# A delta-rule attention, a mixture of experts and a dense layer on one core: identities added by VectorE, weight splits and counts on GpSimd, the gate at the output's eviction, filler matmuls at two boundaries

## What is computed

```python
# attention: q, k, v of shape (4, 8, 768, 48), beta of shape (4, 8, 768)
k_n = k / (norm(k) + 1e-6)
for t in range(768):
    y[:, :, t] = q[:, :, t] @ state
    v_old = state.T @ k_n[:, :, t]
    state += beta[t] * outer(k_n[:, :, t], v[:, :, t] - v_old)
x = y, heads side by side                       # 3072 x 384
# mixture of experts, 8 experts, 1024 hidden
e = argmax(x @ w_gate); p = softmax(x @ w_gate)
out = p[e] * sigmoid(x @ w_output_gate)[e] * (relu(x @ w1[e]) @ w2[e])
# dense layer, 768 hidden
h = max(x @ w1, x @ w2, x @ w3); result = h @ w_out
```

## Time and profile before

| | us |
|---|---|
| median of three runs | 1106.98 (1105.72 to 1110.40) |
| the profiled execution | 1101.72 |
| its span in the profile | 1100.0 |
| TensorE busy | 1019.6 (93%) |
| VectorE busy | 519.5 (47%) |
| ScalarE busy | 366.4 (33%) |
| GpSimd busy | 311.3 (28%) |

### The profile page before, as it was taken

The page is one execution under the profiler, slowest core; times in us unless marked ns, Lnnn a source line. Parts: engine busy times, 40 slices in busy tenths (PEclk is TensorE's granted clock), DMA queues, the critical chain, the costliest instruction groups (busy, mean ns, idle before and its releaser), DMA issues. The chain is left out here.

```text
span 1100.0 us, 30946 instructions
## 1 busy us (share of the span) xinstructions
PE 1019.6 (93%) x13260; PEld 889.7 (81%) x13260; DVE 519.5 (47%) x1134; ACT 366.4 (33%) x731; POOL 311.3 (28%) x202
## 2 busy tenths in 40 slices
PE   4898998999999999849999999998699999999998
PEld 3787887888888888738999999997488888888888
DVE  5566666677666665425444444433342423233221
ACT  1455545455555555412222222221221222122111
POOL 3333242334233423015452555524400001000000
PEclk9999999999999999959999999999699999999999
DMA  9312112121212111045343445223201010100000
GB/s 304 122 34 65 55 41 73 55 72 41 72 56 72 41 45 34 16 172 177 100 149 134 172 172 172 79 86 122 65 22 44 15 44 16 48 18 18 19 11 29
DMA packets 58055, 84.90 MB, mean 77 GB/s; under 512 B 28880, under 2 KB 52816, under 8 KB 55376
## 3 DMA queue, kind: packets, MB, share of 16 engines
q1 hardware_dynamic: 52272, 46.94, 13.5%
q0 software_dynamic: 5664, 36.18, 9.7%
HBM read 61.67 MB, written 21.43 MB: 76 GB/s over the span
## 5 line engine op out<-in xcount | busy, mean ns | idle before, releaser
L1081 PE MATMUL hb<-early,last_h 128*128 128x512 f32 x648 | 207.8, 402 | 1.2 <-DVE early L1213 1.2
L1081 PEld LDWEIGHTS hb<-early,last_h 128*128 128x128 f32 x648 | 121.5, 190 | 29.3 <-DVE early L1213 1.6
L1081 PE MATMUL hb<-early,last_l 128*128 128x512 f32 x324 | 129.1, 399 | 0.0
L1219 DVE TENSOR_TENSOR m<-hb,m 128x512 f32<-128x512 f32 x36 | 24.9, 692 | 132.0 <-PE hb L1081 132.0
L329 PEld LDWEIGHTS bank<-t,n_hi 64*64 64x64 f16 x2688 | 65.2, 110 | 24.7 <-issue 8.9
L541 DVE TENSOR_TENSOR p<-bank,cf 128x512 f16<-128x512 f32 x96 | 66.0, 688 | 30.2 <-PE bank L329 29.2
L329 PE MATMUL bank<-t,n_hi 64*64 64x64 f16 x2688 | 72.2, 195 | 6.0 <-issue 5.2
L1081 PE MATMUL ob<-wo_h,early 128*128 128x384 f32 x288 | 75.1, 339 | 0.0
L1081 PEld LDWEIGHTS hb<-early,last_l 128*128 128x128 f32 x324 | 61.6, 190 | 15.0
L1003 POOL TENSOR_TENSOR late<-w_raw,late 128x3072 fp32r<-128x3072 f32 x8 | 54.5, 6811 | 57.7 <-DVE late L943 57.4
L912 ACT CAST ht_h<-ht_bank 128x512 fp32r<-128x512 f32 x56 | 32.9, 587 | 109.3 <-PE ht_bank L866 55.4
(11 more groups left out here) (163 smaller groups left out, 2213.7 us busy)
## 6 DMA issues: line engine op xcount, KB each, us to landing
w_raw<-w POOLq DMA_DIRECT2D x14, 1536.0 KB, 7.4
kq_t<-qh SPq DMA_DIRECT2D x24, 256.0 KB, 3.3
y_sorted<-y_sb SPq DMA_DIRECT2D x31, 192.0 KB, 1.9
x_in<-x_sorted SPq DMA_DIRECT2D x29, 192.0 KB, 2.9
k_raw<-kt_in SPq DMA_DIRECT2D x24, 192.0 KB, 3.2
v_in<-vh SPq DMA_DIRECT2D x24, 192.0 KB, 3.3
k_own<-kh SPq DMA_DIRECT2D x24, 192.0 KB, 3.1
out<-o_sb SPq DMA_DIRECT2D x24, 192.0 KB, 1.8
```

Source lines behind the costliest of these rows:

```text
L1081: ins = pe.matmul(out, a[x], b[y], start=first and i == 0, stop=last and i == 2, skip_group_check=True)
L1219: dve.tensor_tensor(m1[f % 2][:], h_bank[f % 2][1][:, :], m0[f % 2][:], ALU.max).then_inc(m1_out, 1)
```

## The change

It has five parts.

1. The identity leaves TensorE. The jacobi steps multiply with `n_base`, which is N cut to its 4 x 4 blocks, and VectorE adds the identity as it evicts; the residual's identity is also added at the eviction, which moves from ScalarE to VectorE, and it adds twice the identity, so that "inv" is one group of 16 products instead of two.
2. GpSimd makes `n_base` (new, in the "split" slot), the first expert's weight split (norm parts 10 to 13) and the running count. To this end kn and the mask stand one slot later, and the parts of NORM are spread anew.
3. Twelve matmuls whose result nobody reads stand at the end of attention's TensorE stream, and twelve at the start of the experts'.
4. In the last layer the gather's rows are transposed as they are, the first block's transposes use two banks, and the gate is applied by VectorE as it evicts the output (ScalarE did this before, without a gate).
5. Twelve such matmuls stand at the start of the last layer, and three behind each of the first four transposes.

```diff
-    cf[:, CF_BASE:CF_BASE + C] = (row >> 2 == col >> 2) & (row >= col)
+    cf[:, CF_BASE:CF_BASE + C] = row >> 2 == col >> 2
+    cf[:, CF_EYE:CF_EYE + C] = row == col
+    cf[:, CF_TWO:CF_TWO + C] = 2.0 * (row == col)
...
-    PRE = {-5: ["kn"], -4: ["mask"]}
+    PRE = {-4: ["kn"], -3: ["mask"]}
...
-    NORM = {1: [0], 2: [1], 3: [2], 4: [10], 5: [3], 6: [4], 7: [5], 8: [6], 9: [7, 8], 10: [9], 12: [11], 14: [12]}
+    NORM = {1: [0], 2: [1], 3: [2, 10], 5: [3], 6: [4], 7: [5], 8: [6, 13], 9: [7, 8, 9], 14: [11], 15: [12]}
...
-                    pe.wait_ge(n_hi_ready[st], k + 1)
+                    pe.wait_ge(n_base_ready[st], k + 1)
...
-                diagonal(ident16, ident_rep, pb, True)
-                each_head(n, eye if lv == 0 else t, pb).then_inc(jacobi_done[st], 1)
+                each_head(nb, eye if lv == 0 else t, pb, first=True).then_inc(jacobi_done[st], 1)
...
-                diagonal(ident16, ident_rep, pb, True)
-                diagonal(neg16, flat(t16[st]), pb, False)
+                diagonal(neg16, flat(t16[st]), pb, True)
...
-                each_head(t, eye, ttb, first=True)
                 pe.wait_ge(resid_out[st], k + 1)
                 pe.sem_inc(passed_pe, 1)
-                each_head(pr, tt, ttb).then_inc(inv_done[st], 1)
+                each_head(pr, tt, ttb, first=True).then_inc(inv_done[st], 1)
...
+        for _ in range(12):
+            pe.matmul(bank[1][2][:, :], tri16, flat(n_hi[1]), start=True, stop=True, skip_group_check=True)
...
-                dve.tensor_tensor(t16[st][:], pb, mask_of(None), ALU.mult).then_inc(jacobi_out[st], 1)
+                dve.tensor_tensor(t16[st][:], pb, of_heads(CF_EYE), ALU.add).then_inc(jacobi_out[st], 1)
+            elif what == "resid":
+                dve.wait_ge(resid_done[st], k + 1)
+                dve.tensor_tensor(p16[st][:], pb, of_heads(CF_TWO), ALU.add).then_inc(resid_out[st], 1)
...
+            elif what == "split":
+                pool.wait_ge(gram_out[st], 2 * k + 2)
+                pool.tensor_tensor(n_base[st][:], n_kb_a[par][st][:, :, 0, :], of_heads(CF_BASE), ALU.mult).then_inc(n_base_ready[st], 1)
...
                 pool.wait_ge(slot_ready[st], k + 1)
+                pool.wait_ge(counted_ready, to + 1)
+                pool.tensor_tensor(counted[:], counted[:], chosen[:, to, :], ALU.add).then_inc(counted_ready, 1)
...
+        pe.wait_ge(weights.hi_ready[0], 1)
+        for _ in range(12):
+            pe.matmul(h_bank[1][:, :], w1s[0][0][:, 0, 0:P], w1s[0][0][:, 0, 0:512], start=True, stop=True, skip_group_check=True)
         transpose_x(0)
...
+        keep_warm(12)
         for t in range(NT):
             transpose_x(0, t)
-        for split in weights.last_lo:
-            pe.wait_ge(split, 1)
+            keep_warm(3)
...
+        def output(n, t):
+            dve.wait_ge(o_done, NT * n + t + 1)
+            dve.wait_ge(o_sent[t % 2], 8 * (NT * n + t - t % 2) + 1)
+            dve.tensor_scalar(o_sb[t % 2][:], o_bank[t % 2][:, 0:X], gate[:, bass.ds(NT * n + t, 1)], None, ALU.mult).then_inc(o_out, 1)
```

More of the change, by code:

```diff
@@ L49 @@
 CH_REP = CH_NEG + P
-CH_TRI = CH_REP + U * C
+CH_TRI = CH_REP + C
 CH_ONE = CH_TRI + P
@@ L76, in constants @@
     ch[:, CH_NEG:CH_NEG + P] = -np.eye(P)
-    ch[:, CH_REP:CH_REP + U * C] = np.tile(row == col, (1, U))
+    ch[:, CH_REP:CH_REP + C] = row == col
     ch[:, CH_TRI:CH_TRI + P] = np.arange(P)[:, None] < np.arange(P)[None]
@@ L130, in attention_and_router @@
     n_lo = single("n_lo", [P, U, C], F16)
+    n_base = single("n_base", [P, U, C], F16)
     t16 = single("t16", [P, U, C], F16)
@@ L342, in eye @@
         def eye(s, u):
-            return ident_rep[s, 0:C]
+            return eye16[s, :]
         def inv(k, par, st, what, lv):
             tb, ttb, pb = bank[st]
-            n, nl, t, tt, pr = (lambda s, u, x=x[st]: x[s, u, :] for x in (n_hi, n_lo, t16, tt16, p16))
+            n, nl, nb, t, tt, pr = (lambda s, u, x=x[st]: x[s, u, :] for x in (n_hi, n_lo, n_base, t16, tt16, p16))
             if what == "kt":
@@ L728, in norm @@
                 pool.tensor_tensor(ksq[:], keys, keys, ALU.mult).then_inc(squares, 1)
+            elif part in (10, 11, 12, 13) and 2 <= k < 2 + PIECES:
+                if k == 2 and part == 10:
+                    for i in range(2):
+                        pool.wait_ge(weights.raw_in[i], 16)
+                cols = slice((k - 2) * KX * F // PIECES, (k - 1) * KX * F // PIECES)
+                i = {10: 0, 11: 0, 13: 1, 12: 1}[part]
+                if part in (10, 13):
+                    hi, lo = first_split[i]
+                    ins = pool.tensor_copy(hi[:, cols], weights.flat_raw(i)[:, cols])
+                    if k == 1 + PIECES:
+                        ins.then_inc(weights.hi_ready[i], 1)
+                    else:
+                        ins.then_inc(piece_done, 1)
+                else:
+                    if k == 1 + PIECES:
+                        pool.wait_ge(weights.hi_ready[i], 1)
+                    else:
+                        pool.wait_ge(piece_done, 2 * (k - 2) + 1 + i)
+                    hi, lo = first_split[i]
+                    ins = pool.tensor_tensor(lo[:, cols], weights.flat_raw(i)[:, cols], hi[:, cols], ALU.subtract)
+                    if k == 1 + PIECES:
+                        ins.then_inc(weights.lo_ready[i], 1)
         run(lambda a, c, b, n: walk(a, c, b, n, inv, chain, norm))
@@ L1043, in last_layer @@
     rows = [sb(f"rows{t}", [P, X]) for t in range(NT)]
-    scaled = [sb(f"scaled{i}", [P, X]) for i in range(2)]
     w1_early, w2_early = weights.split_early()
@@ L1082, in three, with x_bank @@
         return ins
+    def x_bank(n, t):
+        return o_bank[t % 2 if isinstance(n, int) and n == 0 else 0]
     def of_blocks(eng, body):
@@ L1131, in transpose_x @@
         def transpose_x(n, t, now=None):
-            pe.wait_ge(scaled_ready, NT * n + t + 1)
-            if t > 0:
-                pe.wait_ge(x_lo, NT * n + t)
-            elif now is not None:
-                pe.wait_ge(o_out, NT * now + 1)
+            pe.wait_ge(rows_got[t], 16 * n + 16)
+            if now is None:
+                to = o_bank[t % 2]
+                if t >= 2:
+                    pe.wait_ge(x_lo, t - 1)
+            else:
+                to = o_bank[0]
+                if t > 0:
+                    pe.wait_ge(x_lo, NT * n + t)
+                else:
+                    pe.wait_ge(o_out, NT * now + 1)
             for c in range(KX):
-                ins = pe.transpose(o_bank[0][:, P * c:P * c + P], scaled[t % 2][:, P * c:P * c + P], ident)
+                ins = pe.transpose(to[:, P * c:P * c + P], rows[t][:, P * c:P * c + P], ident)
             ins.then_inc(x_done, 1)
@@ L1164, in body, with keep_warm @@
                 ins.then_inc(o_done, 1)
+        for split in weights.last_lo:
+            pe.wait_ge(split, 1)
+        def keep_warm(count):
+            for _ in range(count):
+                pe.matmul(h_bank[1][2][:, :], ws[0][0][:, 0, 0:P], ws[0][0][:, 0, 0:512], start=True, stop=True, skip_group_check=True)
+        keep_warm(12)
         for t in range(NT):
             transpose_x(0, t)
-        for split in weights.last_lo:
-            pe.wait_ge(split, 1)
+            keep_warm(3)
         of_blocks(pe, body)
@@ L1191, in body @@
                 split_h(n, f)
-            for t in range(NT):
-                act.wait_ge(o_done, NT * n + t + 1)
-                act.wait_ge(o_sent[t % 2], 8 * (NT * n + t - t % 2) + 1)
-                act.copy(o_sb[t % 2][:], o_bank[t % 2][:, 0:X]).then_inc(o_out, 1)
         for t in range(NT):
@@ L1227, in body @@
             for f in range(KF):
-                if more and f < NT:
-                    scale(n + 1, f)
                 hidden(n, f)
@@ L1232, in body @@
                     x_part(n + 1, f, 1 - par)
+            for t in range(NT):
+                output(n, t)
         for s in range(2):
@@ L1237, in _ @@
         for t in range(NT):
-            scale(0, t)
             x_part(0, t, 0)
```

62 lines of the change are left out of this document (16 added, 46 removed).

## The result

The changed kernel takes 1137.1 us (median of 4 runs, 1128.9 to 1139.6), the kernel before 1107.0 beside it: ratio 1.026, 95% interval 1.021 to 1.030, about 29 us slower where 30 us faster was forecast. The profiled execution took 1139.6 us (span 1137.9).

A forecast was written before the change was run, and what follows sets the result against it. TensorE, busy 93% of the span, was taken as the bound, with dead or slow time around the boundaries. Attention -23, first boundary -1 and second -6 sum to -30 us, from 1107.0 to 1077 us, range 1067 to 1090.

The forecast's parts named there:

- attention term: Attention stage: removed TensorE work and a saved wait, less what waits give back, gain 23 us, ends -12 and -33.
- Removed work: TensorE in attention: identity products and those opening "inv" go, 1.16 us a tile, 27.8 us over 24 tiles.
- n_hi's wait: Attention, ahead of jacobi 0: GpSimd's n_base replaces ScalarE's late n_hi, ending TensorE's wait in one stream, 5 us gained.
- Turn: Attention, after the last jacobi: TensorE waits longer for VectorE's eviction, 24 x 0.22 = 5 us lost.
- Rank: Router in attention: rank waits for five small VectorE operations that do not get shorter, 0.35 us a step, 4 us lost.
- rival D: Attention: GpSimd is late with n_base, slowed beside VectorE, both streams wait, 32 us eat the gain; chance 0.03.
- First boundary: Attention to experts: fillers delay the start but raise the clock for the first expert matmuls; -1 us, ends -2.5 and +2.
- Second boundary: Experts to last layer: earlier first matmul and no half clock in the first group; -6 us, ends -2 and -7.
- B: Attention: slots end on VectorE evictions, half of the 27.8 us comes back, attention gains 11, kernel 1089 us; chance 0.20.
- C: Both boundaries: the fillers do not hold the clock, total gain 24.5 us, kernel 1082.5 us; chance 0.13.

The follow-up runs named there:

- e9: The changed kernel with GpSimd's two weight-piece subtractions moved from slots 14 and 15 into its idle time at slots 10 and 11: 1109.2 us.
- e1: The changed kernel with two thrown-away 64x512 products at each of the four places per tile where the identity's stood: 1110.7 us.
- e5: The changed kernel with 16 thrown-away narrow 64x64 products at each of the four places per tile where the identity's wide pair stood: 1136.2 us.
- e10: The changed kernel with the thrown-away wide products at all four places and the two subtractions moved early on GpSimd: 1101.2 us.
- e3: The changed kernel without any of the filler matmuls at the two boundaries: 1140.4 us.
- e7: The kernel before, with its identity added by 16 narrow 64x64 products instead of two wide 64x512 ones at the same four places: 1123.9 us.
- e4: The changed kernel with attention as in the kernel before, both boundaries and the last layer staying as changed: 1104.5 us.
- e12: Old attention with new boundaries, the residual's wide identity having 2 on its diagonal, so 16 narrow products a tile are left out: 1094.2 us.

## Why the prediction was wrong

**The step that failed** is the attention term, -23 us, and in it what I never costed: that TensorE's clock might not stay at full speed once 24 x 1.16 us of its work was gone. I read 1.00 in the earlier trace rows as a given of the stage, and looked at the clock at the two boundaries alone, though the earlier trace rows shows it falling where TensorE is busy half of the time. Attention's clock went from 0.99 to 0.88, and that alone is up to 52 us. Two things brought it down. One is the rank's wait for a score that GpSimd held up (e9: 43 us less at half clock, 27 us less time, by moving two subtractions); the other is the stream without wide products (e1 against e5). Mending either brings the kernel back to the time before (ratios 1.001 and 1.002) and mending both to 0.995 (e10), so their worths overlap and do not add.

Term by term:
- **Removed work, -27.8.** Nearly right in size: 2.3 us a step forecast, 2.0 of TensorE's busy time found (34.77 to 32.73), and 1.96 of time in e9's best step. Over the whole of e9's attention, though, the gain at full clock is 12 us and not 23. In the changed kernel most of it came back as waits.
- **n_hi's wait, -5.** Right: 5.2 us of waits went. In the ramp TensorE waited 2.2 us for n_base where it had waited 1.5 for n_hi; n_base took 1270 ns where I had taken 1154 from n_lo.
- **Turn, +5.** All waits for t grew by 4.4 us (7.0 to 11.4), the right size, but by the trace only 1.4 us of it stands ahead of the turn (3.5 to 4.9 us); the rest stands ahead of the other jacobi steps, for which I had no term. Nor had I one for the waits for p, 3.4 us.
- **Rank, +4.** 6.3 us, but by another mechanism: I let the five small VectorE operations keep their lengths, and one of them grew from 0.23 to 2.4 us beside GpSimd. With these waits gone (e9) the rank waits 4.4 us, no more than before (4.7), so my own mechanism gave nothing. My reason against rival D, that VectorE's remaining large operations read PSUM, looked past the small ones with two SBUF inputs. The row for it was there, the 1.81 us subtraction.
- **Stops without instructions.** No term. 17.4 us before, 28.0 after; back at 13 with the wide products (e1, e10).
- **The clock.** No term: up to 52 us of attention's time, of which e9 gives back 21 with the four long rank waits gone, and e10 the rest but the tail.
- **First boundary, -1.** 0.1 us from the totals to the first expert matmul, and the experts at full clock from the start took 269.9 instead of 271.2 us: 1.4 together.
- **Second boundary, -6.** 6.6. The fillers' part of it is 2 (e3).

Of the rivals, B had the direction (waits take the work back), but its price, 12 us, was a sixth of the 69 us that attention came out above its forecast. C fell: the clock was back right behind the twelve fillers. D's engine was in it, the other way round: TensorE waited only once for GpSimd's n_base, VectorE did wait for GpSimd's port. A rival in which the clock falls in attention was missing, and with it the chance on "slower" was 0.03 where it should have been several times that.

What stays open: why TensorE runs out of instructions more often, and for up to 3.2 us, when its stream has few wide products (e1 and e5 differ so, 13.2 and 26.9 us, but e7's 19.5 us are no more than the 20.4 of e4 with its wide products; two wide products take 0.22 us and 16 narrow ones 0.28 with eight times the instructions, but that this is the reason was not tested); and how much of the half clock in e9 is due to these stops, since they can't be taken away by themselves.

## What to carry to other kernels

Where the clock can fall as TensorE's did here, work taken off the engine has two prices: its duration and what it did for the clock. Read the granted clock of a stage as a quantity that the change can move, with a chance on it, and test by putting the removed work back as thrown-away work. Before moving work to GpSimd, list every VectorE instruction with two SBUF inputs on the critical chain, however small, and ask what two GpSimd instructions in a row do to it; idle time of GpSimd elsewhere is the place for the rest. And take away narrow matmuls first: e12 left out 16 a tile, kept the wide ones, and was the better for it by 10 us (e4 to e12).

## What was not expected of the hardware

- A VectorE operation on 128x8 with two SBUF inputs took 2.43 us (0.23 alone) across two GpSimd operations back to back (1.14 and 1.46 us); it was not let in between them.
- TensorE stops in the middle of groups of like products without a semaphore, for 0.9 to 3.2 us in the sixteen longest cases of the two kernels, and goes on 1.2 to 1.5 us after a transfer of the instruction queue has ended. The Trainium skill ("Runtime: NRT & Kernel Launch", section "Instruction fetch mechanics") has the fetch hidden behind the issue of instructions; the traces here differ: 9 to 20 us of stops in attention in the nine kernels with all wide products, 20 to 34 in the eight with fewer.
- In the 17 profiles I counted TensorE's idle times in attention (us 40 to 470, outside half clock) and the falls that start from 2 us before to 4 us after their end. Of 91 of 1.3 us and more (a bound of the count alone) 62 have a fall at them, of 241 of 0.5 to 0.9 us 18, and of the 79 between 21. In the nine kernels with all wide products there are 25 of the long ones, with 10 falls; in the eight with fewer, 66 with 52. Of kernels with the changed attention alone, e1 and e10 have 3 long ones and no fall, the seven others 64 with 50. So wide products go with two things: fewer long idle times, and fewer falls at one.
